# Attention scores as fp32 products on two halves of the array, weights turned by transposes

## What is computed

```python
batch, n_heads, seq, head_dim = (4, 8, 576, 64); top_k = 32
scores = scale * np.matmul(q, k.transpose(0, 1, 3, 2))
kth = np.partition(scores, -top_k, axis=-1)[..., -top_k:-top_k + 1]
scores = np.where(scores >= kth, scores, -1000000000.0)
attn = np.exp(scores - np.max(scores, axis=-1, keepdims=True))
attn = attn / (np.sum(attn, axis=-1, keepdims=True) + 1e-09)
x = np.matmul(attn, v)                       # to rows of 512 = heads * 64
h = x @ w_in;  x = (h - np.tanh(h)) @ w_out              # 512 -> 2048 -> 512
h = x @ w_in2; out = np.where(h > 0, h, np.exp(np.minimum(h, 0)) - 1) @ w_out2
```

## Time and profile before

| | us |
|---|---|
| median of 3 runs | 1331.24 |
| the profiled execution | 1331.56 |
| its span, first to last instruction | 1329.6 |
| first 24 slots (9.24 to 142.74) | 133.5 |
| slots 24 to 142 (142.74 to 823.07) | 680.3 |
| rest of the first layer (823.07 to 912.67) | 89.6 |
| second layer (912.67 to 1329.6) | 416.9 |

### The profile page before, as it was taken

One profiled execution on the slowest core, in us unless ns is written; L12 is line 12 of the kernel. 1 busy time (PEld: TensorE's weight loads), 2 busy tenths in 40 slices (PEclk: granted clock), 3 DMA queues, 4 the chain that ended last, 5 costly groups with the idle time before them and its releaser, 6 DMA issues.

```text
span 1329.6 us, 23605 instructions
## 1 busy us (share of the span) xinstructions
PE 1261.2 (95%) x8168; PEld 1052.1 (79%) x8168; DVE 857.1 (64%) x1831; ACT 767.6 (58%) x1771; POOL 588.4 (44%) x966
## 2 busy tenths in 40 slices
PE   3777899999999999999999999999999999999998
PEld 2565688888888888888888888887888888888886
DVE  5988888888888888888888889144542222222221
ACT  5777688777778767778867777343432222222221
POOL 4676466655566654556755555201222222222221
PEclk9867999999999999999999999999999999999999
DMA  6230022100122001013000010045001001010000
GB/s 187 89 109 32 22 63 58 28 17 13 29 60 77 18 18 29 13 49 82 25 16 28 13 29 2 33 143 174 1 1 64 0 0 64 1 48 1 0 32 17
DMA packets 52772, 56.05 MB, mean 42 GB/s; under 512 B 9136, under 2 KB 35760, under 8 KB 52656
## 3 DMA queue, kind: packets, MB, share of 16 engines
q1 hardware_dynamic: 52656, 54.55, 13.6%
HBM read 45.09 MB, written 9.44 MB: 41 GB/s over the span
## 4 chain that ended last, share of the span: by engine, by line
PE 84%; POOL 5%; ACT 4%; issue 3%; DVE 2%; SPq 1%; POOLq 0%; DMA 0%; ACTq 0%; DVEq 0%
PE ps L552 15%; PE ps L521 15%; PE ps L569 15%; PE ps L504 13%; PE ps L465 9%; PE ps L484 7%; PE ps L467 4%; PE ps L453 4%; PE ps L454 2%; POOL kT_hi_over_lo L913 2%; ACT scores L631 1%; POOL gT_lo L952 1%; POOL xT_lo L925 1%; SPq L338 1%; ACT kT_hi_over_lo L604 1%
## 5 line engine op out<-in xcount | busy, mean ns | idle before, releaser
L806 DVE MAX8 best<-work 128x8 f32<-128x576 f32 x432 | 310.3, 746 | 0.1
L1010 POOL TENSOR_TENSOR elu_lo<-elu_h,elu_hi 128x512 fp32r<-128x512 f32 x72 | 93.0, 1291 | 378.9 <-ACT elu_hi L604 378.9
L815 DVE MATCH_REPLACE8 work<-best,work 128x576 f32<-128x576 f32 x288 | 213.9, 743 | 0.0
L879 DVE TENSOR_SCALAR exp_h<-exp_h 128x512 f32<-128x512 f32 x72 | 30.8, 428 | 257.1 <-ACT exp_h L755 257.1
L806 DVE MAX8 best<-scores 128x8 f32<-128x576 f32 x144 | 109.3, 759 | 107.1 <-ACT scores L626 107.0
L465 PE MATMUL ps<-ident,scores 128*128 128x128 f32 x1152 | 163.4, 288 | 5.3 <-POOL ident L943 5.3
L504 PE MATMUL ps<-xT_hi,w_in_hi 128*128 128x256 f32 x576 | 163.4, 284 | 1.4 <-POOL xT_lo L925 1.4
L504 PE MATMUL ps<-xT_hi,w_in_lo 128*128 128x256 f32 x576 | 162.5, 282 | 0.0
L504 PE MATMUL ps<-xT_lo,w_in_hi 128*128 128x256 f32 x576 | 162.1, 281 | 0.0
L755 ACT ACTIVATE exp_h<-ps 128x512 f32<-128x512 f32 x72 | 43.0, 598 | 203.8 <-PE ps L552 203.8
L465 PEld LDWEIGHTS ps<-ident,scores 128*128 128x128 f32 x1152 | 150.4, 202 | 8.8 <-POOL ident L943 8.8
(11 more groups left out here) (77 smaller groups left out, 2930.7 us busy)
## 6 DMA issues: line engine op xcount, KB each, us to landing
kT_raw<-kT SPq DMA_DIRECT2D x64, 144.0 KB, 2.8
qT_raw<-qT SPq DMA_DIRECT2D x128, 64.0 KB, 2.3
w_in_raw<-w_in SPq DMA_DIRECT2D x8, 1024.0 KB, 5.0
w_out_raw<-w_out SPq DMA_DIRECT2D x8, 1024.0 KB, 5.5
ffn_rows<-y_rows SPq DMA_DIRECT2D x18, 256.0 KB, 2.6
v_rows<-v SPq DMA_DIRECT2D x16, 256.0 KB, 2.9
rows<-ffn_rows SPq DMA_DIRECT2D x4, 1024.0 KB, 6.0
out<-out_rows SPq DMA_DIRECT2D x16, 256.0 KB, 2.4
```

The source lines that it names most:

```text
L806: nc.vector.max(best[:, u.t % 3, 1 + n * EIGHT:1 + (n + 1) * EIGHT], src).then_inc(done, 1)
L815: nc.vector.match_replace(wk[:, u.t % 2, :], best[:, u.t % 3, 1 + n * EIGHT:1 + (n + 1) * EIGHT], src, LOWEST).then_inc(chain if n < 2 els ...
L1010: nc.gpsimd.tensor_tensor(g2_lo[:, f % 2, :], g2[:, f % 2, :], g2_hi[:, f % 2, :], ALU.subtract).then_inc(g2_split, 1)
```

## The change

- Scores are fp32 products of the raw q and K. K lies in two halves of its columns, columns 0 to 287 on rows 0 to 63 and 288 to 575 on rows 64 to 127; q lies on both. A head unit is four products over 64 rows and of 144 columns, in the order half 0, half 1, half 0, half 1. A tail unit is eight such products, 64 query columns each. All splitting of q and K goes, and the blanking of q.
- K has two buffers, so the next batch is loaded early; q has a ring of 4; the scores have 5 buffers.
- GpSimd multiplies the exponentials by 1/sum in place (`norm`, 128x576) where it wrote the diagonal matrix (128x128).
- Turning is five transposes of 128 columns against the fixed identity. The last one takes keys 448 to 575, so its first 64 rows repeat keys that chunk 3 holds; V has zeros there, and `attend` uses 128 rows in all five chunks.
- ScalarE's order: `copy_scores` stands right behind `exp_scores`, and `copy_x` behind that.

```diff
-    QRING = 3
+    QRING = 4
+    SCORES = 5
@@ K loads
-        first = last_unit_of[b * PER - 1] - (H - 1)
+        first = 24 if b == 1 else last_unit_of[(b - 1) * PER - 1] + 4
...
-        z = place("kT_hi_over_lo", [P, H, S], F32R)
-        k_up = place("kT_hi_upper", [P, S], F32R)
-        vals = place("v_rows", [P, FULL, PAIRS, 2 * D])
-        q_hi, q_lo, q_raw = place_split("qT", [P, QRING, 2 * P])
-        sc = place("scores", [P, 4, S])
+        keys = place("kT_halves", [P, 2, H, HALF])
+        vals = place("v_rows", [P, FULL + 1, PAIRS, 2 * D])
+        q = place("qT_twice", [P, QRING, 2 * P])
+        sc = place("scores", [P, SCORES, S])
@@ TensorE, scores
-                pe.wait_ge(q_split, n + 1)
+                pe.wait_ge(q_in[n % QRING], (n // QRING + 1) * 2 * DMA)
                 after(pe, copied, u.t)
-                for half in (0, 1):
-                    for i, (slot, head) in enumerate(parts):
-                        rhs = z[:, head, half * HALF:(half + 1) * HALF]
-                        lhs = slice(slot * P, (slot + 1) * P)
-                        pe.matmul(ps[:, half, 0:HALF], q_hi[:, n % QRING, lhs], rhs, start=(i == 0), stop=False)
-                        mm = pe.matmul(ps[:, half, 0:HALF], q_lo[:, n % QRING, lhs], rhs, start=False,
-                                       stop=(i == len(parts) - 1))
+                for part in (0, 1):
+                    cs = slice(part * HALF // 2, (part + 1) * HALF // 2)
+                    for e in (0, 1) if u.tail else (0,):
+                        for half in (0, 1):
+                            rows = slice(half * D, half * D + D)
+                            if u.tail:
+                                mm = pe.matmul(ps[e * D:(e + 1) * D, half, cs], q[rows, n % QRING, e * D:(e + 1) * D],
+                                               keys[rows, buf, 2 * u.pair + e, cs], start=True, stop=True)
+                            else:
+                                mm = pe.matmul(ps[:, half, cs], q[rows, n % QRING, place_ * P:(place_ + 1) * P],
+                                               keys[rows, buf, u.head, cs], start=True, stop=True)
@@ TensorE, turn_weights
-                pe.wait_ge(diag_set, u.t + 1)
+                pe.wait_ge(normed, u.t + 1)
                 for c in range(FULL):
-                    pe.matmul(ps[:, B_TURN, c * P:(c + 1) * P], w[:, c * P:(c + 1) * P], diag[:, :],
-                              start=True, stop=True)
-                pe.matmul(ps[0:REST, rest_bank(u), REST_AT:BANK], w[:, FULL * P:S], diag[:, :],
-                          start=True, stop=True).then_inc(turned, 1)
+                    pe.transpose(ps[:, B_TURN, c * P:(c + 1) * P], w[:, c * P:(c + 1) * P], ident[:, :])
+                pe.transpose(ps[:, rest_bank(u), REST_AT:BANK], w[:, S - P:S], ident[:, :]).then_inc(turned, 1)
@@ ScalarE, the slot
-                if done and done.ends_pair:
-                    copy_x(done)
                 if old:
                     cut_scores(old)
                 if s - 1 in h_in:
                     g_high_part(h_in[s - 1])
                 if old:
                     exp_scores(old)
+                if new:
+                    copy_scores(new)
                 if done and done.ends_pair:
+                    copy_x(done)
...
-                if new:
-                    copy_scores(new)
                 if exped_u:
                     copy_turned(exped_u)
-                for n in q_load_slot.get(s, ()):
-                    if n >= QRING:
-                        q_high_part(n)
-                if s in k_slot:
-                    k_high_part(*k_slot[s])
@@ GpSimd
-            def set_diag(u):
+            def norm(u):
                 po.wait_ge(inverted, u.t + 1)
-                after(po, turned, u.t)
-                nc.gpsimd.tensor_scalar(diag[:, :], ones_at[:, :], rinv[u.t % 2], None, ALU.mult).then_inc(diag_set, 1)
+                w = sc[:, u.t % SCORES, :]
+                nc.gpsimd.tensor_scalar(w, w, rinv[u.t % 2], 1.0, ALU.mult, ALU.mult).then_inc(normed, 1)
```

More of the change, by code:

```diff
@@ L162, in build @@
         ident = place("ident", [P, P])
-        diag = ident
-        ones_at = place("diagonal_ones", [P, P], U8)
         xt_at = at[0]
@@ L442, in scores @@
                 n, place_ = q_of[u.t]
-                pe.wait_ge(q_split, n + 1)
+                pe.wait_ge(q_in[n % QRING], (n // QRING + 1) * 2 * DMA)
+                buf = u.batch % 2
                 if not u.tail:
-                    pe.wait_ge(k_lower, u.batch * H + u.head + 1)
-                    pe.wait_ge(k_split, (u.batch * H + u.head + 1) * 2)
+                    pe.wait_ge(k_in[buf][u.head], (u.batch // 2 + 1) * 2 * DMA)
                 after(pe, copied, u.t)
-                parts = [(place_, u.head)] if not u.tail else [(0, 2 * u.pair), (1, 2 * u.pair + 1)]
@@ L476, in attend @@
                 for c in range(FULL + 1):
[L477 removed]
                     for half in (0, 1):
[L479 removed]
                         if u.tail:
[L481 removed]
+                            weights = pt[:, u.t % 2, c, half * D:(half + 1) * D]
                         else:
[L483 to L485 removed]
+                            weights = pt[:, (u.t - 1 + half) % 2, c, :]
+                        mm = pe.matmul(ps[half * D:(half + 1) * D, B_OUT, cols],
+                                       vals[:, c, u.pair, half * D:(half + 1) * D], weights,
+                                       start=(c == 0), stop=(c == FULL))
                 mm.then_inc(attended, 1)
@@ L604, in high @@
                 return nc.scalar.activation(out_, in_, ACT.Copy)
-            def q_high_part(n):
-                sc_e.wait_ge(q_in[n % QRING], (n // QRING + 1) * 2 * DMA)
-                if qgroups[n][0].tail:
-                    sc_e.wait_ge(q_blank, sum(g[0].tail for g in qgroups[:n + 1]))
-                high(q_hi[:, n % QRING, :], q_raw[:, n % QRING, :]).then_inc(q_high, 1)
-            def k_high_part(b, h):
-                sc_e.wait_ge(k_in[h], (b + 1) * 2 * DMA)
-                after(sc_e, k_split, (b * H + h) * 2)
-                high(k_up[D:P, :], z_raw[D:P, h, :]).then_inc(k_high, 1)
-                high(z[0:D, h, :], z_raw[0:D, h, :]).then_inc(k_lower, 1)
             def w_high_part(n):
@@ L624, in copy_scores @@
                 sc_e.wait_ge(scored, u.t + 1)
[L625 to L626 removed]
+                after(sc_e, turned, u.t - SCORES + 1)
+                nc.scalar.activation(sc[:, u.t % SCORES, :].rearrange("p (a s) -> p a s", a=2), ps[:, 0:2, 0:HALF],
                                      ACT.Copy, scale=SCALE).then_inc(copied, 1)
@@ L820, in invert @@
                 ve.wait_ge(summed, u.t + 1)
-                after(ve, diag_set, u.t - 1)
+                after(ve, normed, u.t - 1)
                 nc.vector.reciprocal(rinv[i], sums_eps[i]).then_inc(inverted, 1)
@@ L968, in _ @@
                 if turned_u:
-                    set_diag(turned_u)
-                    if turned_u.t == T - 1:
-                        po.wait_ge(turned, T)
-                        nc.gpsimd.tensor_copy(ident[:, :], ones_at[:, :]).then_inc(ident_set, 1)
-                for n in q_load_slot.get(s - 1, ()):
-                    if n >= QRING:
-                        q_low_part(n)
+                    norm(turned_u)
                 for n in w_slot.get(s - 1, ())[:1]:
```

113 lines of the change are left out of this document (26 added, 87 removed).

## The result

The changed kernel takes 1205.5 us (median of 4 runs, 1204.3 to 1209.4) where the kernel before takes 1331.7 (4 runs, 1328.9 to 1332.2): a ratio of 0.906, 95% interval 0.9035 to 0.9087. It is 126 us faster. The profiled execution took 1209.37 us with a span of 1207.6.

What follows compares the result with a forecast made beforehand. The prediction took TensorE to bound the kernel, with VectorE's 4.89 us a slot as the floor. From 1331.6 us it took 17 (start), 88 (steady slots) and 4 (end): 1222.6, given as 1222, range 1207 to 1290.

Steps and rivals of the forecast that it cites:

- The scores, the term without a row: TensorE's score products, row halves side by side: 0.79 us behind an `attend`, 0.87 behind `y_step`, 0.24 more than before on average.
- The end: Slots 143 to 146: the four last turnings and attends save 4 us; nothing changes from there on.
- Loads in a row: Rival for the scores: loads of the two row halves follow each other, 46 us more, 1264 us; chance 0.13.
- no overlap: Rival for the scores: the row halves don't overlap at all, 69 us more, 1286 us; chance 0.13.
- dear transposes: Rival for turning: each transpose costs 0.275 us, 0.83 more a slot, 1318 us; chance 0.04.
- exposed loads: Slower rival for the scores: no load is prefetched in the 64-row shape, 1381 us; chance 0.06.
- waits of today included: Slots 24 to 142: TensorE's time put at 587 us, 680.3 less 93, keeping the old kernel's waits.
- I add 5: Slots 24 to 142: 5 us added because level TensorE and VectorE can't absorb each other's hiccups, giving 592.
- from `invert` to the transposes: GpSimd's `norm`, put at 2.0 us, sits on this path: `invert` done 0.95 us into the slot, `norm` at 2.95.
- The start: First 24 slots: slot 24 begins at 125.8 us, 17 less than 142.74.
- for waits at the low clock: First 24 slots: 2.4 us added to 123.4, since products take twice as long at the low clock.
- The floor reached at once: Steady slots: VectorE's floor of 582 us is reached at once, 1209 us in all; the lower end, without its own chance.

Runs made afterwards that it cites:

- e6: The changed kernel with its five transposes written as five plain fp32 products against the identity: 1273.6 us.
- e9: The changed kernel with the last chunk of `attend` over 64 rows again instead of 128: 1215.0 us.
- e10: The changed kernel with all score products on rows 0 to 63 of the array, so the halves can't run side by side: 1274.6 us.
- e4: The changed kernel with the score products in the order half 0, half 0, half 1, half 1: 1205.3 us.
- e7: The changed kernel with two more multiplications of 512 columns on GpSimd ahead of each `norm`: 1226.9 us.
- e12: The changed kernel with one more multiplication of 512 columns on GpSimd ahead of each `norm`: 1206.0 us.
- e14: The changed kernel with four score buffers and ScalarE's old order (`copy_x` first, `copy_scores` behind `tanh_step`): 1223.0 us.
- e3: The changed kernel with the fourth MAX8 over 288 of 576 columns and one of three `y_step` products left out: 1150.6 us.

## Why the prediction came out as it did

**The costs of TensorE were right.** Turning came to 0.46 + 0.09 = 0.55 us, as forecast, and e6 loses 0.55 a slot. `attend` saves 0.15 (e9: 9.5 us for the whole kernel). The scores, the term without a row, take 0.69 and 0.10 of the next product, and behind `y_step` 0.10 of its last product too: 0.79 and 0.89, where 0.79 and 0.87 stood, against 1.28 or so behind an `attend` if e10's mode had held. The end saved 4.0 us, where 4 stood. Loads in a row, no overlap, dear transposes and exposed loads all fell by the rows above; "no overlap" would have given 1286 by the prediction and e10 gives 1275. (The 1318 of the dear transposes takes off 3 us of play where the rivals ahead of it take 5; nothing hangs on it.)

**What failed are two terms in the steady slots: "waits of today included" in the 587, and "I add 5" to a sum that was already at VectorE's floor.** The forecast put TensorE at 587, VectorE at 582, and then 592; measured were 582.3, which is VectorE's floor (119 x 4.882 = 581) and 1.4 us more. 9.7 of the 16.5 us between forecast and median are here, half of them from each term.

The first: the saving of 93 us was right, but it was taken from a time with waits in it that did not stay. Counted from start to start over slots 24 to 142, the parts of TensorE's list exceed their usual lengths by 8 us in the kernel before: `h_step` has 1.75 to 1.92 us in five slots where 1.42 is usual, the turning 1.45 to 1.57 in ten where 1.35 is, and in slot 24 `attend` starts 4.0 us behind the turning's start. In e4's execution they exceed them by 2. Without these waits TensorE has 672 us of work before and 579 in e4, 93 less. So its own sum was 581 (at 4.887 a slot) and not 587. Which part of the change removed which wait isn't shown.

The second: the allowance was given for two level engines that can't absorb each other's waits, with `x_low_part` ahead of a long `norm` inside it. `norm` stood at 2.0 us, taken from the cost of a column in a row of another shape and source type; it measured 0.75, below both prices that the prediction gave (1.4 and 2.0) and below "at least 0.8 added": 0.14 us were added. e7 shows that the place was right, since at 2.24 us the slots behind `x_low_part` lose 6.7 us; at 1.5 us (e12) and at 0.75 nothing is lost, and the 5 us did not arise. That e7, at 1226.9, lies near the forecast of 1222 is in part luck: 9.6 of its 21 us fall in the first 24 slots, where the prediction saw no such cost. The prediction's path "from `invert` to the transposes" was also not the one that held: `norm` stands behind `difference` and the tanh, and in the slot at 489.99 it ended 2.5 us in (491.71 + 0.76), only 0.5 ahead of the forecast's 2.95, although it is 1.25 us shorter.

**The start** was 3.2 us too dear: slot 24 begins at 122.62. The 2.4 us "for waits at the low clock" did not arise. VectorE is busy 115.24 of 115.35 us there at a clock of 0.78, and the price of one slot, 4.8 to 4.9 us, holds from the start. Most of the 18 us that these slots lost don't come from ScalarE's order or the fifth buffer, since e14, which has neither, takes 118.8 there. What the splitting of q and K, the second K buffer and the fourth q pair did for them isn't shown; no run takes them back.

**The profiled execution** was the third part. The sum landed on 1222.3 of it, and 9.7 + 3.2 make it the 1209.4 that it took; the median is 3.9 lower. The windows tell in part why: from 798.80 to 802.20 TensorE's clock is 0.50, that is 1.2 GHz, behind a stretch (790.50 to 798.80) in which it was busy 6.07 of 8.30 us. The second layer takes 417.1 us with it and 414.7 in e4's execution without it, whose span is 5.0 us shorter. Another 10 us, from 122.9 to 133.1, are at 0.50 as well: three slots take 0.9 us more there, and another 0.5 goes in eight slots around the `attend`s of the tail units, which have 4.88 in e4. Why the clock is low in these stretches in some executions and not in others stays open.

**The range** was short by 1.5 us because its lower end was VectorE's floor set against one execution (1209), with 2 us below it. "The floor reached at once" is exactly what came, and it stood as the edge of the range, not as the likeliest case. With TensorE's sum within 1% of the floor of an engine that the change doesn't touch, the floor should have had a chance of its own.

**Priced at nothing, and wrongly:** ScalarE's order and the fifth buffer. Together they are worth 17 us against e14; had only the order been taken over, the kernel would stand at 1294.8. The prediction's sum was not hurt, since the pair of them does what it assumed (nobody waits), but it gave no row for it.

No version here that computes the same beats the changed kernel by more than the runs can tell. e3 shows what is left: both engines would have to lose work.

## What to carry to other kernels

When the sum for one engine comes out within 1% of the floor of another, forecast the floor, don't carry the old kernel's waits over unasked, and price the waits between them only where an engine in the chain is nearly full; check the stretches with extra work (here the splitting of the weights at the start) first. A copy may move ahead in an in-order queue only when the buffer that it overwrites has been released by then: look up what its wait counts on before moving it, and give it one buffer more. A price per column taken from an operation of another type or shape can be wrong by a factor of 2.7; keep both ends of it in the range.

## What the runs showed of the hardware

- A multiplication by a column and a constant on GpSimd, fp32 in place, takes 0.75 us at 128x576, 1.3 ns a column, while the one from uint8 at 128x128 takes 0.61: no common price per column.
- fp32 products on the two row halves overlap whatever their order in the list: pairs start 7 ns apart when they alternate and 13 to 14 when they are grouped, and from the first of the eight records to the next product it is 0.69 and 0.70 us. On one row half it is 1.17 (e10).
- A transpose of 128 fp32 columns starts 0.11 us behind the last one (490.06 to 490.49 for four), and its record lasts 0.27 us (L456). The Trainium skill's "TensorE: Matmul & The Clock Gate", Part 4, has about 275 ns in a kernel's context: that is near the length of a record here, not what one more transpose costs in a row of them. The granted clock stays at 1.00 through the steady slots outside the first ten us (133.10 to 704.93), with five transposes in each.
- A change of the array's shape between two products costs about 0.10 us: 0.22 for the first product behind the scores where 0.12 is usual, 0.33 for the last one ahead of them where 0.23 is.
